# One wait of the matmul queue moved ahead of 48 matmuls at the seam of two stages

## What is computed

```python
# attention: batch 4, heads 8, 576 tokens, head size 64
q_rot, k_rot = rotate(q), rotate(k)
scores = 1/sqrt(D) * q_rot @ k_rot.T
attn = softmax(scores);  x = attn @ v          # -> 2304 tokens x 512
# gated layer, d_ff 1536
x = (sigmoid(x @ w_gate) * (x @ w_val)) @ w_out
# SoLU layer, d_ff 1024
h = x @ w_in;  s = h * softmax(h)
out = (s - mean(s)) / sqrt(var(s) + 1e-6) * g_ln @ w_out
```

## Time and profile before

| | us |
|---|---|
| median of three runs | 971.44 |
| the three runs | 970.36, 971.44, 973.27 |
| the profiled execution: time | 973.27 |
| the profiled execution: span | 971.5 |
| PE busy | 941.3 (97%) |
| PE weight loads busy | 788.7 (81%) |
| DVE, ACT, POOL busy | 507.8, 361.0, 343.0 |

### The profile page before, as it was taken

The page is one execution under the profiler, slowest core; times in us unless marked ns, Lnnn a source line. Parts: engine busy times, 40 slices in busy tenths (PEclk is TensorE's granted clock), DMA queues, the critical chain, the costliest instruction groups (busy, mean ns, idle before and its releaser), DMA issues.

```text
span 971.5 us, 15365 instructions
## 1 busy us (share of the span) xinstructions
PE 941.3 (97%) x5392; PEld 788.7 (81%) x5392; DVE 507.8 (52%) x889; ACT 361.0 (37%) x778; POOL 343.0 (35%) x250
## 2 busy tenths in 40 slices
PE   2899999999999999999999999999999999999998
PEld 1788888888877789888888888888888888888886
DVE  4789889898973524233233233234434454444441
ACT  2778878787772211111110110110111243333332
POOL 5565756556402641500500500600774522222200
PEclk9999999999999999999999999999999999999999
DMA  4233323333230120100200100100111011000001
GB/s 124 62 90 96 85 76 91 82 91 85 73 103 1 65 66 1 66 1 1 65 1 1 65 1 0 43 0 0 43 46 41 0 22 23 22 22 22 22 22 44
DMA packets 32130, 42.78 MB, mean 44 GB/s; under 512 B 5728, under 2 KB 20448, under 8 KB 32096
## 3 DMA queue, kind: packets, MB, share of 16 engines
q1 hardware_dynamic: 32096, 42.32, 15.6%
HBM read 28.74 MB, written 4.72 MB: 34 GB/s over the span
## 4 chain that ended last, share of the span: by engine, by line
PE 93%; DVE 2%; issue 1%; DMA 1%; ACT 1%; POOL 1%; SPq 0%; POOLq 0%; DVEq 0%
PE ps L1065 30%; PE ps L1100 15%; PE ps L1163 10%; PE ps L1002 9%; PE ps L1047 8%; PE ps L1138 8%; PE ps L1029 8%; PE ps L973 2%; PE ps L1148 2%; DMA raw_w<-in_moe_w_out 1%; DMA g_sb<-in_moe_g_ln 0%; DVE qT L791 0%; POOL x_lo L654 0%; DVE nmax L817 0%; POOL w_lo L549 0%
## 5 line engine op out<-in xcount | busy, mean ns | idle before, releaser
L1065 PE MATMUL ps<-x_hi,w_hi 128*128 128x512 f32 (+1 forms) x480 | 177.1, 369 | 0.2 <-POOL w_lo L549 0.2
L1065 PE MATMUL ps<-x_lo,w_hi 128*128 128x512 f32 (+1 forms) x480 | 176.7, 368 | 0.0
L1065 PE MATMUL ps<-x_hi,w_lo 128*128 128x512 f32 (+1 forms) x480 | 176.6, 368 | 0.0
L884 DVE TENSOR_TENSOR hid<-ps,sig 128x512 f32<-128x512 f32 (+1 forms) x60 | 38.3, 638 | 234.7 <-PE ps L1065 206.8
L733 ACT ACTIVATE sig<-ps 128x512 f32<-128x512 f32 (+1 forms) x60 | 33.3, 555 | 295.0 <-PE ps L1065 295.0
L1002 PE MATMUL ps<-kT,qT 128*128 128x288 f32 (+2 forms) x672 | 124.9, 314 | 7.8 <-ACT prob L694 5.1
L817 DVE TENSOR_REDUCE nmax<-ps 128x1 f32<-128x576 f32 x144 | 108.7, 755 | 26.8 <-PE ps L1002 22.9
L593 POOL TENSOR_SCALAR w_hi<-raw_w 128x1024 fp32r<-128x1024 f32 x15 | 41.3, 2777 | 210.5 <-PE ps L1100 210.5
L694 ACT ACTIVATE prob<-ps,nmax 128x576 f32<-128x576 f32 x128 | 94.2, 739 | 51.5 <-DVE nmax L817 50.1
L1002 PEld LDWEIGHTS ps<-kT,qT 128*128 128x128 f32 x672 | 96.0, 194 | 16.9 <-issue 7.4
L1065 PEld LDWEIGHTS ps<-x_hi,w_hi 128*128 128x128 f32 x480 | 90.5, 189 | 16.1 <-issue 0.9
(11 more groups left out here) (109 smaller groups left out, 1638.6 us busy)
## 6 DMA issues: line engine op xcount, KB each, us to landing
kT<-kT SPq DMA_DIRECT2D x30, 288.0 KB, 4.0
raw_k<-in_k SPq DMA_DIRECT2D x16, 288.0 KB, 2.8
raw_q<-in_q SPq DMA_DIRECT2D x16, 288.0 KB, 3.1
out_y<-y_sb SPq DMA_DIRECT2D x36, 128.0 KB, 2.3
v_sb<-in_v SPq DMA_DIRECT2D x64, 64.0 KB, 2.3
raw_w<-in_moe_w_gate SPq DMA_DIRECT2D x6, 512.0 KB, 3.7
raw_w<-in_moe_w_val SPq DMA_DIRECT2D x6, 512.0 KB, 4.7
raw_w<-in_moe_w_out SPq DMA_DIRECT2D x6, 512.0 KB, 6.4
```

The lines of the kernel that those rows point to most:

```text
L884: nc.vector.tensor_tensor(hid[:, f, 0:n], gv_ps[f][1][:, 0:n], sig[:, f, 0:n], ALU.mult).then_inc(hid_ready, 1)
L1065: last = nc.tensor.matmul(in_parts(gv_ps[f][n][:, 0:size(c)], c), w, x, start=m == 0, stop=m == len(todo) - 1)
```

## The change

In the first group PE now waits for all three weight pieces (w_ready 3) at the group's start, as it does in every other group, so ahead of the gate and value matmuls of chunk 1. Before, it waited for the third piece only behind them, ahead of the products of chunk 0. Nothing else differs.

```diff
             def group(gp, u, begun=False):
 
                 i = gp * (2 * CHUNKS) + u * CHUNKS
-                if not begun:
-                    pe.wait_ge(w_ready, gp * 6 + (u * 3 + 3))
+                pe.wait_ge(w_ready, gp * 6 + (u * 3 + 3))
                 order = chunk_order(gp, u)
                 for n, c in enumerate(order):
                     if n > 0 or not begun:
                         gates(i + n, c, u)
-                    if begun and n == 1:
-                        pe.wait_ge(w_ready, 3)
                     if n > 0:
                         products(i + (n - 1), order[n - 1], u, buf(u, n - 1))
                 products(i + (CHUNKS - 1), order[-1], u, buf(u, CHUNKS - 1))
```

## The result

The change makes the kernel slower: 978.41 us (median of five runs, 975.9 to 979.44) against 971.22 before (970.36 to 973.27). The ratio is 1.0067, 95% interval 1.0047 to 1.0088, so +4.6 to +8.5 us. The forecast was 978.4 with a range of 975.8 to 981.6. The profiled execution has a time of 979.1 and a span of 977.3, 5.8 more than the span before.

The account below looks back on a forecast made before the run. The prediction took the kernel as a PE queue with little air, PE busy for 941.3 of 971.5 us. A stall of 5.30 plus 1.7 for the clock, 7.0 us, on the median 971.44 gave 978.4, range 975.8 to 981.6.

Parts of the forecast that it names:

- The view: PE's queue behind the change has almost no waits, 0.14 us idle in 644.89, so what is late stays late.
- First term: PE's first chunk-1 weight load waits for the third w_lo and starts at 327.33 instead of 322.03: 5.30 us.
- Neighbours: Moving the 48 chunk-1 matmuls beside other engines' work gives nothing back and costs nothing: 0, with 0.2 us either way.
- Second term: The clock falls to half in the new PE gap and the 48 matmuls start slow: 1.7 us, band 0.9 to 2.6.
- The total: Stall of 5.30 plus clock term of 1.7 makes 7.0 us over the median of before, 971.44: 978.4.
- (a): Rival: the stall ahead of the 48 matmuls without a low clock, 971.44 + 5.3 = 976.7; chance 0.11.
- (b): Rival: the stall with a double low stretch behind it, 971.44 + 5.3 + 3.4 = 980.1; chance 0.13.
- (c): Rival: not slower, the stall is paid back by PE waits downstream; 971.4 at 7 us or more of them; chance 0.03.
- (d): Rival: the moved wait costs nothing because POOL is through before PE arrives, 971.4; chance 0.02.
- The scatter: The low clock at 292.63 us may be absent from some executions; it lost 1.64 us in 16 PV matmuls.

Follow-up runs that it names:

- e5: The changed kernel run once more, unchanged, for a second profile: 977.87 us, ratio 1.0077 to the kernel before.
- e7: The changed kernel with DVE's rounding of the first two weight pieces put behind S6 and S7 instead of S3 and S4: 977.12 us, ratio 1.0066.
- e2: The changed kernel with POOL's third w_lo put ahead of x_lo of the last pair: 970.76 us, ratio 0.9999 to the kernel before.
- e9: The changed kernel with one more POOL subtraction of the same size between x_lo of the last pair and the third w_lo: 980.04 us, ratio 1.0092.
- e3: The changed kernel with 23 matmuls that nobody reads put on PE ahead of the wait: 975.17 us, ratio 1.0043 to the kernel before.
- e8: As e7, with 23 matmuls that nobody reads put on PE ahead of the wait: 975.31 us, ratio 1.0041 to the kernel before.
- e6: The kernel before with DVE's rounding of the first two weight pieces put behind S6 and S7 instead of S3 and S4: 969.98 us, ratio 0.9986.
- e1: The changed kernel, its early wait asking only for w_ready 2, with w_ready 3 waited for behind chunk 1's gates as before: 970.97 us, ratio 1.0000.
- e10: The kernel before with one more POOL subtraction of the same size ahead of the third w_lo: 970.33 us, ratio 1.0003.
- e4: The changed kernel with the wait for w_ready 3 put behind the first 12 of the 48 matmuls: 974.46 us, ratio 1.0035 to the kernel before.

## Why the prediction was right

- **The view.** PE without a wait from the point of the change to the end, so that a stall stays: it held, 0.18 us of idle in 648.
- **First term, 5.30 us.** Measured 5.21 in three profiles (after, e5, e7). The prediction kept POOL's 4.07 us for x_lo and w_lo; beside an idle PE they took 3.98 or 3.99, which is the 0.09 missing. The terms behind it held too: POOL at the same distance behind the last PV group, and 0.05 us from w_lo's end to the load. That POOL's time sets it was shown by e2 (earlier, cost gone) and e9 (2.30 later, wait 2.30 longer).
- **Neighbours, 0.** e3 and e8 have the 48 matmuls behind the same shift at full clock: 10.95 and 10.90 us against 11.01.
- **Second term, 1.7 us.** The drop came in each of the four profiles with the full stall (after, e5, e7, e9), as forecast, and the size was near: the four executions lost 2.0 us on average, and the timed difference of e7 and e8 is 1.8. The picture behind the size was wrong, though. The prediction had one stretch of 3.41 us, all of it under dense work. In three of the four the clock was low for 6.83 us, and in all four it fell inside the gap (3.6 us into it in after, 319.69 to 323.30), so that part of the stretch cost nothing (table below). The two errors work against each other, and that they left about 1.7 us is in part luck.
- **The total.** By the medians the change costs 7.19 us (after), 6.61 (e5) and 7.14 (e7 less e6), against 7.0. That the median of after is the forecast to 0.01 us is luck: e5, the same kernel, has 977.87.
- **Rivals.** (a), no low clock, is what e3 and e8 build: 975.2 and 975.3, not what the change alone did. (b), a double stretch: the low stretch was twice as long in after, e5 and e9, so (b) had the length right, but only 4.0 to 5.3 us of it had PE at work, so it cost 1.88 to 2.49 us, not 3.4; all four losses lie in the forecast's band of 0.9 to 2.6. (c) and (d) fall with the first bullet and with the wait of 5.14 us.
- **The scatter.** The prediction guessed that the low stretch at 292 us belongs to some executions only. In the profiles that keep the gap at 290 us it is 1.33 to 1.60 us long in six (after, e1, e2, e3, e5, e10), with no low clock behind it, and 1.98 to 2.08 us in three (before, e4, e9), with one each time. That it explains the spread of the timed runs was not shown.

The low stretch behind the stall, in us of each profile's own time; the loss is what the 48 matmuls took over 11.01 us:

| profile | clock low from, to | length | of it PE at work | half of that | loss |
|---|---|---|---|---|---|
| after | 323.30, 330.13 | 6.83 | 5.30 | 2.65 | 2.49 |
| e5 | 321.74, 328.57 | 6.83 | 4.93 | 2.47 | 2.31 |
| e7 | 323.41, 326.82 | 3.41 | 2.94 | 1.47 | 1.37 |
| e9 | 325.29, 332.12 | 6.83 | 4.03 | 2.01 | 1.88 |

The Trainium skill has a rule for this size ("TensorE: Matmul & The Clock Gate", section "Terms"): the penalty is about the throttled time times the share of the clock that is missing. The trace agrees only if the throttled time in which PE has no work is left out: as an estimate by the rule, the whole 6.83 us of after would give 3.4 us and the 5.30 us with PE at work 2.65, and the 48 matmuls lost 2.49. Why the loss is a little under half in all four was not tried.

## What to carry to other kernels

A wait costs what is left of its signal's lateness once the work ahead of it is done, so it belongs as late in the queue as its first reader allows: 48 matmuls (11 us) hid a signal 5.2 us late, 12 hid half of it, none hid nothing, and more POOL work was free in one order and paid in full in the other. Where an engine is busy to the end behind the place, as PE is here, take the stall at its full length and add the clock: half of the low time in which the engine has work. Or move the producer: one subtraction put ahead of another made the early wait free.

## What the runs showed of the hardware

- The long gaps of TensorE cost more than their length. Behind 5.14 to 7.44 us without work the clock was at 0.50 (1.2 GHz) in four profiles of four, and the 48 matmuls took 1.4 to 2.5 us more. The clock fell inside the gap and stayed low for 6.83 us in three of them and 3.41 in one. Behind 2.18 us in e4 it stayed at 1.00, behind 1.98 to 2.08 us at 290 us it fell in three profiles of three. The length of a gap of about 2 us alone doesn't tell which.
- 23 matmuls with no reader, in place of the idle time, kept the clock at 1.00, which was worth 1.8 us (e7 against e8). The 5.3 us by which the wait delays PE stayed.
- POOL's x_lo and w_lo together took 3.98 or 3.99 us where PE stood idle beside them (after, e5, e7) and 4.06 or 4.07 where PE worked, on its 48 matmuls (before, e1) or on the filler (e3, e8). What in PE's work does it was not tried.
- POOL's subtraction of 128x1024 with the same tensor as both inputs took 1.89 us and the real one right behind it 2.67, where the real one alone takes 2.33 to 2.40; together they put w_lo off by 2.30 us, which is near one operation. Why the second is longer was not tried.
